# Softmax sums turned on TensorE, inverted as nine rows and written to DRAM in rows of 128

## What is computed

```python
q_pool = q.reshape(2, 8, 576, 2, 64).mean(axis=3)          # pairs of the 1152 query rows are averaged
scores = matmul(q_pool, k^T) / 8                           # 2 batches, 8 heads, 1152 keys
attn = exp(scores - max(scores));  attn = attn / (sum(attn) + 1e-9)
x = concat_heads(matmul(attn, v))                          # 1152 tokens x 512
h = x @ w_in                                               # 512 x 2048
g = (a0 + a1 h + a2 h^2 + a3 h^3) / (1 + |b0||h| + |b1| h^2 + 1e-6)
x = g @ w_out                                              # 2048 x 512
xn = x / rms(x) * rms_g
out = (silu(xn @ w_gate) * (xn @ w_val)) @ w_out2          # 512 x 1536, 1536 x 512
```

## Time and profile before

| | |
|---|---|
| median of the timed runs | 729.79 us |
| the profiled execution, its time | 725.3 us |
| its span in the trace | 723.5 us |
| granted TensorE clock, mean of the span | 0.979 |
| attention, roughly | 0 to 256 us |
| passage from attention to the first MLP | 256 to 319 us |
| both MLPs | 319 to 723 us |

### The profile page before, as it was taken

How to read it: one execution, slowest core, us unless ns; L and a number is a source line. 1 busy time by engine, 2 the same in 40 slices (tenths; PEclk the granted TensorE clock), 3 DMA queues, 4 the chain that set the end, 5 groups by cost and what they waited for, 6 DMA issues and landing times.

```text
span 723.5 us, 11771 instructions
## 1 busy us (share of the span) xinstructions
PE 679.5 (94%) x3931; PEld 630.4 (87%) x3931; DVE 523.4 (72%) x1009; ACT 411.1 (57%) x855; POOL 438.1 (61%) x427
## 2 busy tenths in 40 slices
PE   8999999899989918789999999999999999999998
PEld 5899999798989818679999988989999999999996
DVE  6899998899978814888889988997664444444442
ACT  5787787677868714878888888874521111111110
POOL 5886878689868647698878978965642603000000
PEclk9999999999999967999999999999999999999999
DMA  7684673957565222010011011112130110000012
GB/s 222 187 245 115 168 186 92 245 109 201 125 153 140 50 84 64 11 59 30 30 59 59 1 59 59 58 45 73 59 115 3 59 59 1 0 1 1 1 43 88
DMA packets 33596, 60.76 MB, mean 84 GB/s; under 512 B 12496, under 2 KB 14992, under 8 KB 33424
## 3 DMA queue, kind: packets, MB, share of 16 engines
q1 hardware_dynamic: 33264, 59.87, 29.5%
q10 hardware_dynamic: 288, 0.33, 0.2%
HBM read 43.78 MB, written 2.40 MB: 64 GB/s over the span
## 4 chain that ended last, share of the span: by engine, by line
PE 69%; POOL 11%; DMA 9%; ACT 4%; DVE 3%; issue 3%; SPq 2%; POOLq 0%; ACTq 0%; DVEq 0%
PE hb L829 27%; PE ob L878 21%; PE sc L752 6%; PE sc L760 5%; DMA recip_rows<-recip 4%; PE misc L774 3%; PE tb L829 3%; DMA km_lo<-kqB 3%; PE pv_ps L774 3%; DMA o_part<-o_sb 1%; POOL o_part L596 1%; POOL kqB L523 1%; DMA qrawA<-in_q 1%; POOL v2A L535 1%; POOL qrawB L508 1%
## 5 line engine op out<-in xcount | busy, mean ns | idle before, releaser
L944 ACT ACTIVATE pt_hi<-sc 128x384 fp32r<-128x384 f32 x216 | 90.7, 493 | 55.0 <-PE sc L760 53.7
L1109 DVE TENSOR_REDUCE neg_part<-sc 128x1 f32<-128x384 f32 x216 | 107.7, 549 | 19.2 <-PE sc L752 18.0
L829 PE MATMUL hb<-xt_hi,wi_hi 128*128 128x384 f32 x280 | 96.6, 345 | 21.3 <-POOL xt_lo L613 17.7
L1118 DVE TENSOR_TENSOR pt_lo<-sc,pt_hi 128x384 fp32r<-128x384 f32 x216 | 106.7, 548 | 3.5 <-ACT pt_hi L944 2.6
L878 PE MATMUL ob<-wo_hi,gt_hi 128*128 128x512 f32 x252 | 100.0, 397 | 3.6 <-DVE gt_lo L1193 2.4
L878 PE MATMUL ob<-wo_lo,gt_hi 128*128 128x512 f32 x252 | 99.7, 396 | 0.0
L878 PE MATMUL ob<-wo_hi,gt_lo 128*128 128x512 f32 x252 | 99.5, 395 | 0.0
L829 PE MATMUL hb<-xt_hi,wi_lo 128*128 128x384 f32 x280 | 95.6, 342 | 0.0
L829 PE MATMUL hb<-xt_lo,wi_hi 128*128 128x384 f32 x280 | 95.5, 341 | 0.0
L935 ACT ACTIVATE prob<-sc,neg_max 128x1152 f32<-128x1152 f32 x72 | 89.2, 1239 | 3.1 <-DVE neg_max L1111 3.1
L760 PE MATMUL sc<-ident,prob 128*128 128x128 f32 x648 | 83.9, 275 | 0.7 <-ACT prob L935 0.6
(11 more groups left out here) (159 smaller groups left out, 1706.0 us busy)
## 6 DMA issues: line engine op xcount, KB each, us to landing
wraw<-in_moe_w_out SPq DMA_DIRECT2D x7, 1024.0 KB, 5.0
krawB<-in_k SPq DMA_DIRECT2D x8, 576.0 KB, 4.9
qrawB<-in_q SPq DMA_DIRECT2D x8, 512.0 KB, 6.1
wraw<-in_moe_w_in SPq DMA_DIRECT2D x4, 1024.0 KB, 5.3
krawA<-in_k SPq DMA_DIRECT2D x7, 576.0 KB, 6.0
o_part<-o_sb SPq DMA_DIRECT2D x14, 288.0 KB, 5.5
qrawA<-in_q SPq DMA_DIRECT2D x7, 512.0 KB, 7.8
wraw<-in_moe_w_gate SPq DMA_DIRECT2D x3, 1024.0 KB, 5.0
```

The lines of the kernel that those rows point to most:

```text
L829: ins = nc.tensor.matmul(bank[:, 0:BLOCK], w[i][:, d, col], x[j][:, d, BLOCK * nb:BLOCK * nb + BLOCK], start=d == 0 and n == 0, stop=d == ...
L944: nc.scalar.activation(pt[0][:, 3 * c:3 * c + 3, PT_COL[i]:PT_COL[i] + P], src, ACT.Copy).then_inc(pt_hi, 1)
L1109: nc.vector.tensor_reduce(neg_part[:, s, c:c + 1], sc[s][:, c, 0:KBANK], AX.X, ALU.max, negate=True).then_inc(part_done, 1)
L1118: nc.vector.tensor_tensor(pt[1][:, kt, col], src, pt[0][:, kt, col].bitcast(F32), ALU.subtract).then_inc(pt_lo, 1)
```

## The change

`sums_plus` moves from step i = 2 to step i = 0 on ScalarE. TensorE turns the nine columns of sums with one more turn per head (`turn_sums`), in step i = 2, before `qk` of tile 4, into the unused last 128 columns of the first bank of scores; in the last head twice, in steps 5 and 8. VectorE inverts 9 partitions x 128 from that bank (5 and 4 partitions in the last head), in step i = 3 between the first and the second of the three maxima of tile 4. The write to DRAM then has nine rows of 512 bytes. In SyncE's order B's mixed keys are copied before `load_kq(0)`. GpSimd does the sum, the scaling and the split of two heads in one go (`two_heads`), before it splits B's queries and keys, and splits A's values before B's query parts. Behind attention, VectorE and ScalarE take some small steps in another order.

```diff
-        recip = sbuf(top, "recip", [P, 2, TILES])
+        recip = sbuf(top, "recip", [P, 3, P])
+        def sums_bank(s):
+            return sc[s][:, 0, KBANK:BANK]
             def rows_of_recip(h, par):
-                sp.wait_ge(recip_done, h * 2 + 2)
-                    sp.dma_start(recip_rows[par].rearrange("t p -> p t"), recip[:, par]).then_inc(row_out, 16)
+                sp.wait_ge(recip_done, h + 1)
+                sp.dma_start(recip_rows[par], recip[0:TILES, par]).then_inc(row_out, 16)
             def last_rows(n):
-                sp.wait_ge(recip_done, 2 * PAIRS + 2 * n)
-                    sp.dma_start(recip_rows[1, t0:t1].rearrange("t p -> p t"), recip[:, 1, t0:t1]).then_inc(tail_out[n], 16)
+                sp.wait_ge(recip_done, PAIRS + n)
+                sp.dma_start(recip_rows[1, t0:t1], recip[0:t1 - t0, 1 + n]).then_inc(tail_out[n], 16)
 # SyncE, pair
                 else:
+                    mixed_keys(1, h)
                     sp.wait_ge(k_split[0], h * 2)
                 sp.wait_ge(q_split[0], h * 4 + 4)
                 load_kq(0, h + 1)
-                if not is_first(h):
-                    mixed_keys(1, h)
 # GpSimd
+            def two_heads(h, n):
                 pool.wait_ge(k_split[0], h * 2)
                 pool.wait_ge(shifted, n * 64 + 64)
                 nc.gpsimd.tensor_tensor(o_part[0][:], o_part[0][:], o_part[1][:], ALU.add).then_inc(x_sum, 1)
                 pool.wait_ge(x_sum, n + 1)
                 pool.wait_ge(row_in, n * 32 + 32)
                 nc.gpsimd.tensor_tensor(o_part[0][:], o_part[0][:], r_row[:], ALU.mult).then_inc(x_scaled, 1)
+                pool.wait_ge(x_scaled, n + 1)
                 nc.gpsimd.tensor_scalar(xt[0][:, n], o_part[0][:], 1.0, 0.0, ALU.mult, ALU.add).then_inc(x_hi, 1)
 # GpSimd, split_second_half
-                if n is not None:
-                    scale_rows(n)
-                    pool.wait_ge(x_scaled, n + 1)
                 mixed_sum(h)
+                values_free(0, h)
+                values_hi(0)
+                pool.wait_ge(m_split, h * 4 + 1)
+                mixed_hi()
+                values_lo(0, h)
+                mixed_lo(h)
                 queries_hi(1)
                 queries_lo(1, h)
-                if n is not None:
-                    split_x(n)
 # GpSimd, pair
-                    if batch:
-                        sum_parts(h + 1, n)
-                    split_second_half(h + 1, n if batch else None)
+                    if par == 0 and not is_first(h):
+                        two_heads(h + 1, n)
+                    split_second_half(h + 1)
 # TensorE
+            def turn_sums(bank, par, t0, t1):
+                ins = nc.tensor.transpose(bank[0:t1 - t0], sums_eps[:, par, t0:t1], ident[:])
+                ins.then_inc(sums_t, 1)
+                    if i == 2 and not is_first(h):
+                        pe.wait_ge(sums_done, h)
+                        pe.wait_ge(pt_lo, h * 27 + 7)
+                        turn_sums(sums_bank(s), 1 - par, 0, TILES)
 # ScalarE
-                    if i == 2 and not is_first(h):
+                    if i == 0 and not is_first(h):
                         sums_plus(h - 1, 1 - par)
 # VectorE
-                nc.vector.reciprocal(recip[:, par, t0:t1], sums_eps[:, par, t0:t1]).then_inc(recip_done, 1)
+            def recips(bank, count, slot, t0=0, t1=TILES):
+                dve.wait_ge(sums_t, count)
+                nc.vector.reciprocal(recip[0:t1 - t0, slot], bank[0:t1 - t0]).then_inc(recip_done, 1)
+                    if i == 3 and not is_first(h):
+                        between = lambda: recips(sums_bank(1 - s), h, 1 - par)
+                    if i == 6 and is_last(h):
+                        between = lambda: recips(sums_bank(1 - s), PAIRS, 1, *SUMMED[0:2])
+                    if i == 8 and is_last(h):
+                        recips(sc[0][:, 0, 0:P], PAIRS + 1, 2, *SUMMED[1:3])
                     lo_parts(i, h, s)
 # behind attention, unit u: ScalarE copies pv's last group before last_hi(2);
 # VectorE takes denominator(0) before last_scaled(2), and last_lo(2) in unit 1
```

More of the change, by code:

```diff
@@ L369, in rows_of_recip @@
             def rows_of_recip(h, par):
-                sp.wait_ge(recip_done, h * 2 + 2)
-                with nc.allow_non_contiguous_dma(reason="one number of each row for each of nine tiles"):
-                    sp.dma_start(recip_rows[par].rearrange("t p -> p t"), recip[:, par]).then_inc(row_out, 16)
+                sp.wait_ge(recip_done, h + 1)
+                sp.dma_start(recip_rows[par], recip[0:TILES, par]).then_inc(row_out, 16)
                 sp.wait_ge(row_out, h * 16 + 16)
@@ L380, in last_rows @@
                 t0, t1 = SUMMED[n], SUMMED[n + 1]
-                sp.wait_ge(recip_done, 2 * PAIRS + 2 * n)
-                with nc.allow_non_contiguous_dma(reason="one number of each row for some tiles"):
-                    sp.dma_start(recip_rows[1, t0:t1].rearrange("t p -> p t"), recip[:, 1, t0:t1]).then_inc(tail_out[n], 16)
+                sp.wait_ge(recip_done, PAIRS + n)
+                sp.dma_start(recip_rows[1, t0:t1], recip[0:t1 - t0, 1 + n]).then_inc(tail_out[n], 16)
                 sp.wait_ge(tail_out[n], 16)
@@ L783, in pair @@
                     turn(i, h, s)
+                    if is_last(h) and i == 8:
+                        pe.wait_ge(sums_done, PAIRS + 1)
+                        pe.wait_ge(pt_lo, 27 * PAIRS - 3)
+                        turn_sums(sc[0][:, 0, 0:P], par, *SUMMED[1:3])
                     if i in (0, 1):
@@ L793, in pair @@
                         pv(g, h, j0, j1)
+                    if i == 2 and not is_first(h):
+                        pe.wait_ge(sums_done, h)
+                        pe.wait_ge(pt_lo, h * 27 + 7)
+                        turn_sums(sums_bank(s), 1 - par, 0, TILES)
+                    if i == 5 and is_last(h):
+                        pe.wait_ge(sums_done, PAIRS)
+                        pe.wait_ge(pt_lo, h * 27 + 16)
+                        turn_sums(sums_bank(s), par, *SUMMED[0:2])
                     if i + 2 < TILES:
@@ L949, in sums_plus @@
                 act.wait_ge(exp_done, h * 9 + t1)
[L950 removed]
+                nc.scalar.activation(sums_eps[:, par, t0:t1], sums[:, par, t0:t1], ACT.Identity, bias=eps_bias[:]).then_inc(sums_done, 1)
             def o_copy(g, h):
@@ L1104, in _, with row_max @@
             split_first(dve)
-            def row_max(i, h, s):
+            def row_max(i, h, s, between=None):
                 n = (h * 9 + i) * 3
@@ L1109, in row_max @@
                     nc.vector.tensor_reduce(neg_part[:, s, c:c + 1], sc[s][:, c, 0:KBANK], AX.X, ALU.max, negate=True).then_inc(part_done, 1)
+                    if c == 0 and between:
+                        between()
                 dve.wait_ge(part_done, n + 3)
@@ L1127, in pair @@
                     s = (par + i) % 2
+                    between = None
+                    if i == 3 and not is_first(h):
+                        between = lambda: recips(sums_bank(1 - s), h, 1 - par)
+                    if i == 6 and is_last(h):
+                        between = lambda: recips(sums_bank(1 - s), PAIRS, 1, *SUMMED[0:2])
                     if i + 1 < TILES:
-                        row_max(i + 1, h, 1 - s)
+                        row_max(i + 1, h, 1 - s, between)
                     elif not is_last(h):
                         row_max(0, h + 1, 1 - s)
+                    if i == 8 and is_last(h):
+                        recips(sc[0][:, 0, 0:P], PAIRS + 1, 2, *SUMMED[1:3])
                     lo_parts(i, h, s)
[L1133 to L1136, removed]
             def tokens_lo(t):
@@ L1236, in _ @@
                 if u == 0:
+                    last_scaled(2)
+                if u == 1:
                     last_lo(2)
```

22 lines of the change are left out of this document (6 added, 16 removed).

## The result

The changed kernel takes 707.93 us (706.22 to 710.97, 4 runs) beside 729.5 us before (726.72 to 731.82, 4 runs): the ratio is 0.971, interval 0.9662 to 0.9759. The forecast was 712.5 us and a range of 704 to 720. The profiled execution is the slowest of the four: span 709.2 us, 14.3 less than before. The experiments ran on three chips (e1 to e4, e5 to e8, e9 to e12). The changed kernel and e5 were each timed on two chips and came out within 1 us of themselves (707.93 and 708.85, 697.22 and 697.13); so times of different chips are compared here, but differences of 1 to 2 us are not taken as shown.

A forecast was written before the change was run, and what follows sets the result against it. TensorE, busy 94% of the span, was taken as the bound, so only its gaps, clock and added work count. Removing 26.3 us and adding 9.0 gains 17.3, from 729.8 to 712.5 us, range 704 to 720.

The forecast's parts named there:

- The write: SyncE's write of inverted sums to DRAM: as rows of 512 bytes it takes 2.1 us instead of 10.4.
- The end of attention: Passage to the MLP: first product 14.3 us earlier, ScalarE's second unit 16.5 us earlier, bounds 14.0 to 18.0.
- Middle heads: SyncE gets 8 us back per head; waits on mixed keys, 5.3 us, and ScalarE's late copy, 0.7, go.
- M: The forecast's zero mark in a head: the start of its mixed product on TensorE.
- The inversion: VectorE inverts 128 numbers per partition in 0.8 us, exposed in each head: 4.7 us added, bounds 1.3 to 8.5.
- The term with the turn: Added in the heads: 1.3 us for TensorE's turns and 4.7 us for VectorE's exposed inversion.
- GpSimd's one piece: Two heads in one go: values waits, 3.8 us, go; new mixed-key waits in heads 3, 5, 7 add 3.0 us.
- The sum: Whole kernel: 26.3 us removed, 9.0 added, a gain of 17.3 us.
- the 3.0 us of waits on mixed keys: Heads 3, 5 and 7: TensorE newly waits 1.0 to 1.2 us each for B's mixed keys, bounds 0 and 9.
- Rival (A): The write in rows is no faster, 10 us being a fixed price: 734 us, slower; chance 0.03.
- Rival (C): GpSimd's one piece becomes a wait of 3 us in each batch head, 9 instead of 3: 719 us; chance 0.15.

The follow-up runs named there:

- e1: The changed kernel with SyncE's and GpSimd's orders of the kernel before, so the rows alone with the small moves behind attention: 702.91 us.
- e4: The changed kernel with sums inverted and written in columns as before, the new SyncE and GpSimd orders kept: 745.87 us.
- e5: e3 with VectorE inverting the nine columns before TensorE turns them, then only copying in the old place: 697.22 us.
- e8: e3 with B's mixed keys copied behind `load_kq(0)` again, as in the kernel before: 697.88 us.
- e9: e5 with the last values product of attention ahead of the first MLP product on TensorE: 696.02 us.
- e12: e3 with twelve small DRAM writes behind its end, six forms twice, each waited for: nine columns of 4-byte numbers 9.72 us, nine rows 1.25 us.
- e6: e3 with a second inversion of the same numbers into a tile that nobody reads: 705.04 us.
- e3: The changed kernel with SyncE issuing the shift of the head before ahead of `load_kq(1)` instead of behind `load_v(0)`: 698.86 us.
- e2: The changed kernel with GpSimd's order of the kernel before: 701.99 us.
- e11: The changed kernel timed once more, on the same chip as e5 and e9: 708.85 us.

## Why the prediction was right, and where its steps were not

**The write.** The step was right: the gain is the write's. I took 2.1 us from 256 KB; it is 1.17 us at the end of attention and 1.25 alone. What I had left open, whether the price goes with the bytes, e12 settled: the same 4.5 KB take 9.72 or 1.25 us, by how they lie.

**The end of attention.** I counted 14.3 us at the first MLP product and 16.5 at ScalarE's second unit. The product waits 1.86 instead of 17.72 us, 15.9, and the passage is 19.0 us shorter. At ScalarE's second unit, the point at which I counted, it is 10.0 us behind the end of attention (273.55 - 263.5) instead of the 12.7 of the forecast and the 29.2 before. The term was 2.6 us too small: 1.5 of it is the wait that is left (1.9 instead of 3.4), 0.8 the low clock that I kept for the first unit (3.17 instead of 4.0 us, at a granted clock of 0.70), 0.2 the values product.

**Middle heads.** "SyncE gets 8 us back per head" is right only for the rows without the new orders. In heads 1 to 6 the time from the write's issue to the read back's was 8 to 10.5 us before; it is 2.4 to 3.2 in e1, and 6.2 to 7.8 in the changed kernel (115.47 to 123.26 in the rows above), where the write is issued close behind the bunched loads. In the last head it is 1.7. For GpSimd's one piece I had counted just that (read back issued at M + 9.5; in head 2 at 88.19, 9.6 us after its mixed product at 78.58).

**The inversion.** I had 5 ns a number, 0.8 us. It is 934 ns for 128 and 204 for 9: 6.1 ns a number. The rule of the Trainium skill, VectorE: DVE Perf Modes (section on the 8-slice pipeline), read as eight cycles a number, gave 1.2 us as an estimate; the measured time lies between my slope and it. My working had slips that did not decide: the old inversion stands in the rows with 0.20 us and not 0.12, the bounds 0.3 and 1.4 us give 0.6 and 9.4 us by my own rule and not 1.3 and 8.5, and 1.2 us need 8.1 ns a number and not 8.9. Exposed it is, as e6 shows. The term with the turn was 6.0 us for eight heads; a head of e3 is 29.87 - 29.17 = 0.70 us longer, 5.6.

**GpSimd's one piece.** The step that failed is its last sentence but one, the list of who waits. I expected 1.0 us on the mixed keys in three heads and named SyncE's wait at B's keys "with `load_kq(0)` and all loads behind it", and stopped there. Up to B's keys the count holds: the one piece ends at M + 20.4 (20.7 counted), B's keys at M + 25.6 (25.9 counted). The copy lands in 3.2 us instead of the 4.4 that I took, and the mixed keys are in time. What the list leaves out comes behind: B's query parts, finished 11.8 us after the one piece, at M + 32.2; B's loads, which wait for them; and, one queue entry behind the loads, the shift. For the shift ScalarE waits, in the middle of its loop. The issue of the shift moves by only 1.1 us against e2; the loads bunched ahead of it make its transfer 5.2 us longer. The prediction asks neither what is sent just ahead of the shift nor who needs its buffer.

The price in the profile is 8.8 us of waits and the low clock behind them. I forecast 254.8 us for the end of attention; it is 263.5 in that profile, 259.1 in e11's, and 248.6 in e3's, which takes the cause away and nothing else. The medians of e3 and the changed kernel are 9 us apart. The profiled executions of e3 and e11 are 7.2 us apart (698.99 and 706.22), less than the 10.4 us between their ends of attention, because all behind it took 3.2 us longer in e3; why is open.

**The sum.** 17.3 us were forecast; the medians are 21.6 apart, the profiled spans 14.3. That the total came out well is in part luck; it rests on errors that offset each other. The passage gave more than I counted, the 3.0 us of waits on mixed keys did not come, and the new wait with its low clock was missed. Without the fault attention ends at 248.6 us (e3), 6 us sooner than I forecast; the fault took up that much and more. Rival (A), whose price I had put at 734 us, is e4 at 745.87: that world is slower than the kernel before, as said, by more than counted, as the late shift stands in it as well (11.8 us of ScalarE's waits). Rival (C), a wait of 3 us per head from the one piece, had the right origin and nearly its size in waits (9 us counted, 8.8 measured), but two waits in place of three, no clock behind them, and the wrong path.

## What to carry to other kernels

A small DMA that the issuing engine waits for is priced by that engine's silence, not by its bytes: before the order around it is tuned, look at how it lies in DRAM. Here a turn on TensorE of 0.28 us and an inversion of 0.93 us took the write from 9.7 to 1.25 us (e12). When one piece of work is put ahead on an engine, follow every semaphore that moves with it through the DMA queue to the last entry, and ask of each for whom a buffer comes free, not only whose data arrive. Look at the time to landing beside the time of issue: a transfer issued at nearly the same moment can land 5 us later when the loads ahead of it were held up and leave together. A change whose parts help and hurt can look like a clean gain; each part alone, on the chip, shows what to keep.

## What the runs showed of the hardware

Writes of 4 bytes side by side into one 512-byte line of DRAM took 7.8 us for 128, with no DMA engine busy in the last 6 us, and 9.7 and 11.7 us for 1152 in nine lines, while the same 4.5 KB as 36-byte, 64-byte or 512-byte pieces took 1.2 to 1.7 us (e12). The second half of the shift, 288 KB, landed 9.3 us after its issue when 1.5 MB of loads had been issued within the 2.1 us before the shift, and 4.1 us after it when the last of these loads had been issued 3.8 us before (the changed kernel and e2, head 3). VectorE's inversion took 204 ns for 9 numbers in each partition and 934 for 128, 6.1 ns more for each further number (a copy of the same nine rows took 268 ns in all), whatever the number of partitions (4, 5 or 9: 946, 934, 934 ns); a second one right behind took 0.88 instead of 0.93 us. A wait of 4.7 us on TensorE was followed by 6 us at a granted clock of 0.52, one of 4.0 us by 6.3 us at 0.73 (the changed kernel).
